# Zeros multiplied at the start, high parts first in the first and last step, a store moved to ScalarE's queue, and last copies shared with VectorE

## The reference

```python
# attention, per head, block by block (64 positions), lam[h] about 0.97..0.99
Dmask = np.where(rel >= 0, lam[:, None, None] ** rel[None, :, :], 0.0)
intra = np.einsum('bhic,bhjc->bhij', qb, kb) * Dmask[None]
intra = np.einsum('bhij,bhjd->bhid', intra, vb)
inter = np.einsum('bhid,bhde->bhie', qb * lam_pow[None], kv_state)
out[:, :, sl] = intra + inter
kv_state = lam_block * kv_state + np.einsum('bhsd,bhse->bhde', kb * rev_pow, vb)
# first block: x is (1536, 512), w_in (512, 2048), w_out (2048, 512)
h = x @ w_in;  x = np.maximum(0.01 * h, h) @ w_out
# second block: w1, w2 (512, 1024), w3 (1024, 1024), w_out (1024, 512)
a = x @ w1;  b = x @ w2;  y = ((a * b) @ w3) @ w_out
```

## Time and profile before

| what | value |
|---|---|
| median of 3 runs | 561.89 us (561.79 to 562.08) |
| the profiled execution | 561.46 us |
| its span | 559.5 us |
| PE busy | 548.2 us, 98% of the span |
| DVE, ACT, POOL busy | 197.2, 169.1, 31.0 us |
| slices in which PE is not at 9 tenths or more | the first (5) and the last (6) of 40 |
| DMA, mean busy share in the first six slices of 14 us | 8, 8, 8, 7, 9, 8 tenths |

### The profile page before, as it was taken

How to read it: one execution, slowest core, us unless ns; L and a number is a source line. 1 busy time by engine, 2 the same in 40 slices (tenths; PEclk the granted TensorE clock), 3 DMA queues, 4 the chain that set the end, 5 groups by cost and what they waited for, 6 DMA issues and landing times.

```text
span 559.5 us, 7724 instructions
## 1 busy us (share of the span) xinstructions
PE 548.2 (98%) x2842; PEld 453.8 (81%) x2842; DVE 197.2 (35%) x300; ACT 169.1 (30%) x297; POOL 31.0 (6%) x42
## 2 busy tenths in 40 slices
PE   5999999999999999999999999999999999999996
PEld 4788888788888888888888888788888888888885
DVE  3656875545433322222535453411101111110110
ACT  3336444534423322221424343311112111131112
POOL 5331330000000000000000000000000000000000
PEclk9999999999999999999999999999999999999999
DMA  8887983532311000000012310000001000020002
GB/s 340 296 288 253 332 280 98 170 113 80 110 52 43 0 0 0 0 0 0 19 57 75 114 38 0 1 1 0 1 0 60 15 0 0 0 76 0 1 0 75
DMA packets 18393, 41.79 MB, mean 75 GB/s; under 512 B 1969, under 2 KB 3001, under 8 KB 16833
## 3 DMA queue, kind: packets, MB, share of 16 engines
q1 hardware_dynamic: 17040, 32.00, 16.8%
q10 hardware_dynamic: 1328, 9.45, 4.6%
HBM read 36.19 MB, written 5.25 MB: 74 GB/s over the span
## 4 chain that ended last, share of the span: by engine, by line
PE 96%; DVE 1%; ACT 1%; DMA 1%; issue 0%; SPq 0%; DVEq 0%; ACTq 0%
PE hid L568 16%; PE hid L570 16%; PE hid L569 16%; PE acc L568 15%; PE acc L569 14%; PE acc L570 14%; PE hid L599 2%; PE hid L632 2%; PE hid L626 2%; PE hid L646 1%; DVE g_lo L450 1%; DMA stage<-weights 1%; ACT g_hi L369 0%; ACT g L363 0%; PE hid L608 0%
## 5 line engine op out<-in xcount | busy, mean ns | idle before, releaser
L568 PE MATMUL hid<-xy_hi,wa_hi 128*128 (+1 forms) x384 | 149.6, 390 | 0.2 <-issue 0.2
L570 PE MATMUL hid<-xy_hi,wa_lo 128*128 (+1 forms) x384 | 149.4, 389 | 0.0
L569 PE MATMUL hid<-xy_lo,wa_hi 128*128 (+1 forms) x384 | 149.4, 389 | 0.0
L363 ACT ACTIVATE g<-hid 128x512 f32<-128x512 f32 (+1 forms) x72 | 43.1, 599 | 259.3 <-PE hid L570 259.2
L568 PE MATMUL acc<-g_hi,wb 128*128 128x512 f32 x288 | 112.3, 390 | 0.9 <-DVE g_lo L450 0.9
L569 PE MATMUL acc<-g_lo,wb 128*128 128x512 f32 x288 | 112.1, 389 | 0.0
L570 PE MATMUL acc<-g_hi,wb 128*128 128x512 f32 x288 | 112.0, 389 | 0.0
L568 PEld LDWEIGHTS hid<-xy_hi,wa_hi 128*128 128x128 f32 x384 | 72.1, 188 | 15.6 <-issue 0.8
L570 PEld LDWEIGHTS hid<-xy_hi,wa_lo 128*128 128x128 f32 x384 | 72.1, 188 | 15.1
L569 PEld LDWEIGHTS hid<-xy_lo,wa_hi 128*128 128x128 f32 x384 | 72.0, 188 | 14.9
L512 DVE TENSOR_TENSOR g<-g,hid 128x512 f32<-128x512 f32 (+1 forms) x48 | 33.0, 687 | 120.1 <-ACT g L363 120.1
(11 more groups left out here) (49 smaller groups left out, 311.4 us busy)
## 6 DMA issues: line engine op xcount, KB each, us to landing
stage<-weights SPq DMA_DIRECT2D x80, 256.0 KB, 3.3
qkv<-attn ACTq DMA_DIRECT2D x9, 1024.0 KB, 7.3
qkv<-attn SPq DMA_DIRECT2D x3, 1024.0 KB, 8.6
outT<-stage SPq DMA_DIRECT2D x12, 256.0 KB, 2.0
stage<-w_dram SPq DMA_DIRECT2D x8, 256.0 KB, 2.6
w_dram<-qkv SPq DMA_DIRECT2D x4, 256.0 KB, 2.4
decay<-pow_dram SPq DMA_DIRECT2D x1, 512.0 KB, 4.4
w_dram<-g SPq DMA_DIRECT2D x2, 256.0 KB, 7.6
```

The costliest lines, as they stand in the source:

```text
L363: nc.scalar.mul(g[:, n % 2, :], hid[:, n % 2, 0, :], factor).then_inc(scaled, 1)
L568: nc.tensor.matmul(out, w_hi, a_hi, start=first, stop=False)
L569: nc.tensor.matmul(out, w_hi, a_lo, start=False, stop=False)
L570: return nc.tensor.matmul(out, w_lo, a_hi, start=False, stop=final)
```

## The change

Five edits. (1) DVE first writes zeros into `probs`, and TensorE multiplies them four times (128 by 128 on 256 columns, float32) into a bank that nobody reads, before its first real matmul. (2) Step 0 is written as four matmuls high by high, four low by high, and four high by low, and each group waits only for its own parts. The last step of the kernel begins with the four matmuls of its first two banks that don't need the low part of the hidden tile. (3) The store of the powers moves from SP to ACT, behind the high parts of w0 to w7. (4) SP now waits for that store behind w7, and the loads of chunk 1 and chunk 2 move behind it: chunk 1 behind the load of `decay`, chunk 2 behind w9. (5) In the last copies DVE takes bank 1 and the first half of bank 3, ACT the rest; ACT copies its half of bank 3 after DVE's half, and stores it through its own queue.

```diff
+WARM_UP = 4
+TAIL_HALVES = (slice(0, TOK // 2), slice(TOK // 2, TOK))
...
+        def last_out(d, cols):
+            return outT[d, :, (NT - 1) * TOK + cols.start:(NT - 1) * TOK + cols.stop]
...
@@ sync
-            for c in range(ATTN_RING):
+            def load_chunk(c):
                 sp.dma_start(qkv[:, c, :, :], attn[c]).then_inc(chunk_loaded[c], 16)
-                if c == 0:
-                    for w in range(4, STAGE):
-                        load_weight(w)
-
-            wait_then_step(pow_chain, POW_STEPS)
-            sp.dma_start(pow_dram.ap(), pow_row[:, :]).then_inc(pow_stored, 16)
+
+            load_chunk(0)
+            for w in range(4, STAGE):
+                load_weight(w)
+
             wait_then_step(pow_stored, 16)
             every_shift = bass.AP(pow_dram, 0, [[1, P], [2 * CHUNK, H], [1, CHUNK]])
             sp.dma_start(decay[:, :, :], every_shift).then_inc(decay_loaded, 16)
 
+            load_chunk(1)
             for w in range(STAGE, NW):
                 load_weight(w)
+                if w == STAGE + 1:
+                    load_chunk(2)
...
-            with sp.Fori(0, NT) as t:
+            with sp.Fori(0, NT - 1) as t:
...
+            for d in range(KD_TILES):
+                cols = TAIL_HALVES[0] if d == KD_TILES - 1 else slice(0, TOK)
+                wait_then_step(tail_copied[d], 1)
+                sp.dma_start(last_out(d, cols), stage[:, d, cols]).then_inc(out_stored, 16)
+            wait_then_step(out_stored, 16 * KD_TILES * NT)
+            wait_then_step(tail_stored, 16)
@@ scalar
             for w in range(2 * EARLY_34):
                 weight_hi(w)
+            act.wait_ge(pow_chain, POW_STEPS)
+            act.dma_start(pow_dram.ap(), pow_row[:, :]).then_inc(pow_stored, 16)
...
-            copy_out(NT - 1)
+            for d in (0, 2):
+                act.wait_ge(bank_done, (KD_TILES - 1) * (2 * NT - 1) + d + 1)
+                nc.scalar.copy(stage[:, d, :], acc[:, d, :]).then_inc(tail_copied[d], 1)
+            last, cols = KD_TILES - 1, TAIL_HALVES[1]
+            act.wait_ge(acc_done, CREDIT_G + N1 + F2 * NT)
+            act.wait_ge(tail_copied[last], 1)
+            nc.scalar.copy(stage[:, last, cols], acc[:, last, cols]).then_inc(tail_copied[KD_TILES], 1)
+            act.wait_ge(tail_copied[KD_TILES], 1)
+            act.dma_start(last_out(last, cols), stage[:, last, cols]).then_inc(tail_stored, 16)
@@ vector
+            nc.vector.memset(probs[:, :, :, :], 0.0).then_inc(zeroed, 1)
...
+            dve.wait_ge(out_stored, 16 * KD_TILES)
+            dve.wait_ge(bank_done, (KD_TILES - 1) * (2 * NT - 1) + 1 + 1)
+            nc.vector.tensor_copy(stage[:, 1, :], acc[:, 1, :]).then_inc(tail_copied[1], 1)
+            last, cols = KD_TILES - 1, TAIL_HALVES[0]
+            dve.wait_ge(acc_done, CREDIT_G + N1 + F2 * NT)
+            nc.vector.tensor_copy(stage[:, last, cols], acc[:, last, cols]).then_inc(tail_copied[last], 1)
@@ tensor
-            w34_products(0, HALF)
+            pe.wait_ge(zeroed, 1)
+            for _ in range(WARM_UP):
+                nc.tensor.matmul(hid[:, 1, 0, 0:2 * P], probs[:, 0, 0, :], probs[:, 1, 0:2, :], start=True, stop=True)
+            pe.wait_ge(hi_done, PLACE["wl", 0] + 1)
+            for f in range(HALF):
+                nc.tensor.matmul(acc[:, f, :], w3_ring[:, 0, 0, f * P:(f + 1) * P], g_hi[:, 0, :], start=True, stop=False)
+            pe.wait_ge(split_done, CREDIT_SPLIT + PLACE["w3", 0] + 1)
...
+            pe.wait_ge(split_done, CREDIT_SPLIT + PLACE["wl", 0] + 1)
+            for f in range(HALF):
+                nc.tensor.matmul(acc[:, f, :], w3_ring[:, 0, 0, f * P:(f + 1) * P], g_lo[:, 0, :], start=False,
+                                 stop=False).then_inc(w34_done, 1)
```

More of the change, by code:

```diff
@@ L177, in build @@
         out_stored = sem("out_stored")
+        zeroed = sem("zeroed")
+        tail_copied = [sem(f"tail_copied{i}") for i in range(KD_TILES + 1)]
+        tail_stored = sem("tail_stored")
         def tokens(t):
             return bass.ts(t, TOK)
+        def last_out(d, cols):
+            return outT[d, :, (NT - 1) * TOK + cols.start:(NT - 1) * TOK + cols.stop]
         def dest(name):
@@ L601, in score @@
                 last.then_inc(scored, 1)
-            w34_products(0, HALF)
+            pe.wait_ge(zeroed, 1)
[6 more added lines that the diff above has]
+            for f in range(HALF):
+                nc.tensor.matmul(acc[:, f, :], w3_ring[:, 0, 1, f * P:(f + 1) * P], g_hi[:, 0, :], start=False, stop=False)
+            pe.wait_ge(split_done, CREDIT_SPLIT + PLACE["wl", 0] + 1)
+            for f in range(HALF):
+                nc.tensor.matmul(acc[:, f, :], w3_ring[:, 0, 0, f * P:(f + 1) * P], g_lo[:, 0, :], start=False,
+                                 stop=False).then_inc(w34_done, 1)
             pe.wait_ge(selector_loaded, 16)
@@ L719, in _ @@
                     out_step(t, f)
-            for f in range(F2):
-                if f + 1 < F2:
-                    gates(N1 + F2 * (NT - 1) + f + 1, f + 1)
+            for f in range(F2 - 1):
+                gates(N1 + F2 * (NT - 1) + f + 1, f + 1)
                 out_step(NT - 1, f)
+            n, f = N1 + F2 * NT - 1, F2 - 1
+            pe.wait_ge(g_hi_done, n + 1)
+            for d in range(2):
+                cols = slice(d * P, (d + 1) * P)
+                nc.tensor.matmul(acc[:, d, :], wb[:, f, 0, cols], g_hi[:, f % 2, :], start=False, stop=False)
+                nc.tensor.matmul(acc[:, d, :], wb[:, f, 1, cols], g_hi[:, f % 2, :], start=False, stop=False)
+            pe.wait_ge(g_split, CREDIT_G + n + 1)
+            for d in range(2):
+                cols = slice(d * P, (d + 1) * P)
+                nc.tensor.matmul(acc[:, d, :], wb[:, f, 0, cols], g_lo[:, f % 2, :], start=False,
+                                 stop=True).then_inc(bank_done, 1)
+            for d in range(2, KD_TILES):
+                cols = slice(d * P, (d + 1) * P)
+                last = product(acc[:, d, :], wb[:, f, 0, cols], wb[:, f, 1, cols], g_hi[:, f % 2, :], g_lo[:, f % 2, :],
+                               False, True)
+                last.then_inc(bank_done if d < KD_TILES - 1 else acc_done, 1)
 def source_of(name):
```

## The result

The changed kernel takes 566.25 us (median of 4 runs, 565.13 to 566.87) against 561.96 us before; the ratio is 1.0077 (95% interval 1.0062 to 1.0091). It is slower by 4.3 us, where I had forecast 2.0. The profiled execution takes 565.7 us with a span of 563.7, so 4.2 us more than the 561.46 and 559.5 of before.

What follows compares the result with a forecast made beforehand. TensorE was taken to bound the kernel, holding 96% of the chain of waits. +3.3 us (chunk 1's late mask) - 1.3 (the end) = +2.0 us, so a median of 563.9 us; range 561.2 to 566.2.

Steps and rivals of the forecast that it cites:

- the gate: At L632 of chunk 1: its mask waits on DVE behind w11, so it starts at 32.5 instead of 29.17, costing 3.3 us.
- Behind this gate everything goes on with a fixed order at TensorE's pace: After L632 of chunk 1: later loads cost nothing, and the 3.3 us stay until the end.
- rival (a): Start and new waits: zeros do not raise the pace (565.7), or the pace falls in the waits (2.2 us); chance 0.18.
- My price for 1 MB: Transfers on SP's queue: 1 MB at 422 GB/s takes 2.5 us.
- The first gate: At L632 of chunk 0: mask ready at 21.6 against 22.70 before; TensorE, ready at about 19.9, idles 1.7 us.
- POOL holding up DVE: On chunk 2: DVE's subtraction of w10 takes 1.53 us instead of 0.69 beside POOL, ending at 29.65.
- rival (b): Around w10: POOL does not hold up DVE's subtraction, taking 1.1 us off; 562.8, no measurable change; chance 0.17.
- The zeros: At the start: raise TensorE's pace 4 us earlier, near 6.5; L608 starts at 9.0 instead of 10.96, 2.0 us ahead.
- first form: Rival (a) at the start: zeros do not raise the pace, L608 starts at 10.8, 1.8 us later; 565.7.
- second form: Rival (a) in the new waits of 1.7 to 2.3 us: the pace falls, a slow stretch costing 2.2 us.
- The end: Last step and last copies: last issue moves from 557.0 to 555.7, 1.3 us gained (0.9 to 1.7).
- Rival (c): Transfers of w8 to w11 do not come behind the chunks; w11 by about 23, kernel faster, 559.5; chance 0.13.

Runs made afterwards that it cites:

- e2: The changed kernel, but ACT stores the powers behind the casts of w0 to w3 instead of w0 to w7: 559.15 us, ratio 0.9966.
- e6: The changed kernel, but chunks 1 and 2 are loaded ahead of the wait for the store, as before; store still late on ACT: 559.67 us, ratio 0.997.
- e3: The changed kernel, but SP loads chunk 2 behind w11 instead of behind w9: 560.74 us, ratio 0.9991.
- e7: The changed kernel, but POOL begins with chunk 2 only when DVE has split w11: 564.71 us, ratio 1.0046.
- e8: The changed kernel itself, run again beside other experiments: 565.99 us (563.48 to 566.76, 6 runs), ratio 1.0065.
- e4: The changed kernel, with TensorE multiplying zeros into bank 0 of acc in the two waits of chunk 1: 563.8 us, ratio 1.005.
- e9: The changed kernel with powers stored behind w3's cast and chunk 2 loaded behind w11, but without the four matmuls of zeros: 559.3 us, ratio 0.9958.
- e1: The kernel before, with only the changed kernel's end (last step high parts first, last copies shared): 560.25 us, ratio 0.9978.
- e10: The changed kernel's zeros, step 0 and end, with before's store on SP and before's order of loads: 560.28 us, ratio 0.9981.
- e5: The changed kernel with the powers stored behind w3's cast and chunk 2 loaded behind w11: 558.01 us, ratio 0.9932.

## Why the prediction was right and wrong

The direction was right, and so was the mechanism up to the gate: the store behind four casts (e2 takes that away), the loads behind the store (e6), w11 behind chunk 2 (e3), POOL beside DVE (e7). That DVE's order then passes w11's delay on to the state and the mask of chunk 1 was not changed in any run; it is read from the rows: w11 split at 30.59, the mask ended at 32.71, 2.12 us later, against 2.13 before.

The size was not. The failing step is the sentence "Behind this gate everything goes on with a fixed order at TensorE's pace". It does not: the waits that I had worked out (1.7 to 2.3 us; measured 1.93 and 2.23) lower the clock. In the profile this is 1.6 us behind the gate (4.16 instead of 2.58), in e8's profile 2.8 against e4; between the times it is 0.8 to 2.2 (e4). The forecast had this term at nothing. I had it as a side of rival (a), at 2.2 us, and gave all of (a) 0.18, since the clock had not fallen after the 0.73 us at the end. A wait of 0.73 says nothing on one of 2. With this term in the sum, 3.3 + 1.6 - 1.3 = 3.6 us, the forecast would have been 565.5; the rest is the gate's size.

The other terms:

- The gate: forecast 3.3, measured 3.8. w11 was split 0.24 us later than forecast, and L687 does not start with the mask's end but 0.23 behind it. The forecast went straight from the mask to L632 and left out L626, which needs the state and gates just as late. `decay` was issued at 15.24, 0.6 sooner than my 15.8, since the store landed within 1.4 us instead of 2.1. Chunk 2 landed at 27.1, not 26.6, though everything began sooner: 4.0 us behind w9 (ACT's cast at 23.11) instead of 2.5. My price for 1 MB was too low here. That w10 still came near its forecast (27.68, forecast 27.25) is luck: w9 was in hand by 23.11, 1.0 sooner than forecast, and chunk 2 took 1.5 longer.
- The first gate: I forecast an idle 1.7 us before L687 of chunk 0. There was none; the mask was ready at 20.48 (19.19 + 1.29) and TensorE came at 20.63. The first wait came one step later, for w9 (1.93 us). The forecast had no gate there, though by its own times w9 would have landed at 24.1, when TensorE would have been ready for step 4; it cost nothing, since w11 came later still.
- POOL holding up DVE: forecast to 29.65, measured 29.98 (28.32 + 1.66). Right; rival (b) falls by this row. e7's trace has the subtraction without POOL beside it, at 0.69.
- The zeros: pace up before L651 was through (L651's four start at 5.21, L654 at 6.70, then 0.23 us apart), and L663 at 9.48 instead of 9.0, as POOL ended the powers at 9.34 instead of 8.92. Rival (a) in its first form falls by this and by e9. In its second form, the fall of the pace in the new waits, it is what happened, and its 2.2 us lies between the 1.6 and 2.8 of the profiles.
- The end: forecast 1.3, measured 1.2, and alone 1.2 (e1).
- Rival (c): the tiles came in the order of issue; it falls.

Sum of the profile: 3.8 + 1.6 - 1.2 = 4.2, which is 563.7 - 559.5.

## What to carry to other kernels

When a wait is put on a queue, list all that stands behind it and ask what the transfer engines do meanwhile: here one 8 KB store left them nearly empty for 5 us (11 to 16), and TensorE paid 3.8 us for it, at a tile that was behind a larger load. A new wait of about 2 us on TensorE can have a second price, the slow clock behind it, which was 1.6 and 2.8 us in the two profiles of the changed kernel. It comes in some executions and not in others, so it scatters the times. The spread by itself is no proof, since the kernel before spans 2.8 us (560.12 to 562.88) with mean granted clocks of 0.999 and 1.000; the mean granted clock of each execution, and then the windows, tell. Gains of the same change are told apart by running each alone: the end (1.2 us) and the zeros (0.8 us in the profiles and 1.3 between the medians, once nothing else gates) were real, and with the two orders repaired the kernel is 3.5 to 3.8 us faster than before.

## What the hardware showed that I had not expected

- The length of a wait alone does not decide whether the clock falls. It fell behind TensorE's waits of 0.97 us (e6), 1.73 (e2), 1.93 and 2.23 (changed kernel), 2.23 (e3), 2.52 (e7) and 3.22 (e8), and the granted clock reads 0.50 to 0.66 in the windows on these stretches. It did not fall behind 0.73 (before), 0.89 (e2, for the powers), 1.06 (e1), 1.28 (e10), 2.12 (e7, its first) and 2.20 (e8, its first). Among e2's five executions one has a mean granted clock of 0.996 and takes 561.53, and four have 0.999 or 1.000 and take 559.1 to 559.3. So the same program loses the clock in one execution and keeps it in another.
- An 8 KB store to DRAM on ACT's queue, which held nothing else, let its waiter go 1.4 us after issue when the transfer engines were nearly empty (13.86 to 15.24), and 2.0 to 3.4 us after it when they were at work for SP's queue (e6 14.86 to 16.86, e5 9.18 to 11.40, e2 9.13 to 11.76, e9 8.58 to 12.01). Before, behind 2 MB on the same queue, it took from 9.03 to 16.38. So an empty queue of one's own takes away most of that wait, not all.
- 1 MB behind w9 took 4.0 us to be whole at 385 GB/s (windows of 3 us from 24), where 2.5 would do for its bytes. e4 and e8 show it too (3.9 and 3.7), and e3 with chunk 2 behind w11 (3.7, from 24.37 to 28.06). In e2, with the early store, chunk 2 takes 2.5 (19.78 to 22.30), but w11 is 2.0 behind w10 (22.98 to 25.02) instead of the usual 0.65. Why, no run here tells.
